# Dynamic convolution ahead of a two-layer product: channel blocks on partitions, and VectorE's 32x32 block turn in place of TensorE's transposes

## The chip, the cores and the metric

The kernel runs on one core of a Trainium2 chip. Its metric is the device time of one launch in microseconds (us), the median of three runs. Besides TensorE (PE; its weight loads are shown apart as PEld), VectorE (DVE), ScalarE (ACT), GpSimd (POOL) and SyncE (SP), the trace shows 16 DMA engines. Each engine works through its own instructions in order; semaphores are the only order between engines. TensorE's clock is shown as a share of its full speed.

## What is computed

```python
batch, seq, d_model = (4, 4096, 192)      # x: fp32
kernel_size, n_heads = 7, 8               # weight_gen: (4, 4096, 8, 7)
w = softmax(weight_gen, axis=-1)          # with + 1e-09 in the denominator
x_pad = concatenate([zeros(B, 6, D), x])  # six zero tokens ahead of each sequence
attn = einsum('bshk,bskhg->bshg', w, x_unf)   # seven taps per token and head, 24 channels a head
h = attn.reshape(16384, 192) @ w_in       # w_in: 192 x 2048
g = h * (1 / (1 + exp(-1.702 * h)))
out = g @ w_out                           # w_out: 2048 x 192
```

## The kernel before

**Precision.** Both products take fp32 values as a rounded part ("hi", type fp32r) and what is left of them ("lo"), so each fp32 product is three fp32r ones. The 192 rows of the first product are split into 128 "main" rows and 64 "rest" rows; the rest rows' hi and lo parts are stacked on 128 partitions (`xtr`), so one pass covers both. A 128-wide chunk of the hidden layer takes five matmuls of 512 columns (L474 to L479).

**Tiles.** Partition p holds the 128 tokens from 128p on. A tile takes 4 tokens of each partition (`TT = 4`), 512 tokens in all; there are 32 tiles. The first two and the last two tiles are written out, those between run in a loop of two tiles a turn (`over_tiles`). In each tile the 16 chunks are taken as 8 pairs, m = 0 to 7.

**One pair.** PE: `first_product` (10 matmuls into one of two `hid` slots in PSUM), then `second_product` of two pairs ago (`LAG = 2`, 16 matmuls into `acc`). ACT: `gate` (L268) and `gate_hi` (L271) from `hid`. DVE: `gate_lo` (L402), then the steps of the convolution of a coming tile that the table `CONV_AT` gives this pair. The second product of pair n waits for `gate_lo` of pair n; the first product of pair n waits for `gate_hi` of pair n-2, whose slot it writes.

**Convolution.** 18 steps on DVE: sum, add, reciprocal and product of the softmax on 128 x 32 and 128 x 224, then seven multiplications of 128 x 768 (L320) and six additions (L327; the last is split in `conv`, 128 x 512, and `conv_rest`, 128 x 256, L335). The window `xwin` holds 4 tokens and 6 tokens of halo. The first two windows' halo is loaded from the neighbouring partition's tokens in four DMAs of 31 partitions each (`first_window`, L188); later windows get theirs by an ACT copy from the window before (`carry_halo`, L255, at m = 3).

**Turning the tile.** The convolved tile has tokens on partitions and must have channels there. At m = 6 (`T_AT`) PE does six 128 x 128 transposes with the identity (L445, L448) into a `hid` slot. ACT then reads the rounded parts from it (L236, L238) and DVE the remainders (L371, L375).

**Start.** SP issues all loads in this order: the taps of three tiles, window 0 and its halos, the first layer in two halves of three DMAs, the identity, window 1 and its halos, the second layer, the remaining taps. DVE subtracts the maxima of the first taps, convolves tile 0, rounds the second layer (L365), splits tile 0 and then takes the second layer's remainder (L382). ACT rounds the first layer (L229, L230), POOL takes its remainders in four operations (L429). During tile 0 DVE takes four maxima of the remaining taps (L349), POOL subtracts each (L435), and in tile 1 ACT takes four exponentials, each with two table loads.

**End of a tile.** At m = 1 of the next tile ACT lifts one part of `acc` into `outs` (L248) and DVE adds the other (L391); `second_product` of m = 0 waits for that addition, part by part. SP stores `outs`.

Of the kernel before, what the change touches and what calls it, by code (L numbers as in the profile page):

```python
# [5 lines left out]
P = 128  # L22
# [5 lines left out]

TT = 4
LAG = 2  # L30
# [10 lines left out]
def ffn_of_dynamic_conv(nc: bass.Bass, x: bass.AP, weight_gen: bass.AP, w_in: bass.AP,  # L41
                        w_out: bass.AP, ident_dram: bass.AP, out: bass.AP):
    B, S, D = x.shape
    H, K = weight_gen.shape[2:]
    F = w_in.shape[1]
    GRP = D // H
    HALO = K - 1
    T = B * S // P
    TILES = T // TT
    NTOK = TT * P  # L50
    CH = F // P
    PAIRS = CH // 2
    STEPS = PAIRS + 1
    REST = D - P
    WIN = TT + HALO
    HK = H * K
    BATCH_P = P // B
    assert REST == 64 and NTOK == 512 and CH % 2 == 0 and TILES % BODY == 0 and (STEPS * BODY) % 2 == 0
    assert (BODY * PAIRS) % HI_SLOTS == 0 and S % T == 0


    FIRST_TILES = 3
    FIRST_TOKENS = FIRST_TILES * TT
    SHIFTS = 4
    STEP_TOKENS = (T - FIRST_TOKENS) // SHIFTS
    assert FIRST_TOKENS + SHIFTS * STEP_TOKENS == T
    HALVES = (slice(0, F // 2), slice(F // 2, F))
    TAP_PARTS = [(0, TT), (TT, FIRST_TOKENS)] + [(FIRST_TOKENS + i * STEP_TOKENS, FIRST_TOKENS + (i + 1) * STEP_TOKENS)
                                       for i in range(SHIFTS)]

    x_rows = x.rearrange("b s d -> (b s) d").rearrange("(p t) d -> p t d", t=T)
    out_rows = out.rearrange("b s d -> (b s) d").rearrange("(p t) d -> p t d", t=T) if len(out.shape) == 3 \
        else out.rearrange("(p t) d -> p t d", t=T)
    wg_rows = weight_gen.rearrange("b s h k -> (b s) (h k)").rearrange("(p t) c -> p (t c)", t=T)

    with ExitStack() as ctx:
# [5 lines left out]

# [9 lines left out]
        ident = sb("ident", [P, P])  # L92

        taps = sb("taps", [P, T * HK])
        tap_max = sb("tap_max", [P, T * H])
        tap_sum = sb("tap_sum", [P, TT * H])
        tap_inv = sb("tap_inv", [P, TT * H])
        tap_norm = sb("tap_norm", [P, TT * HK])
        xwin = sb("xwin", [P, 2, WIN, D])
        prod = sb("prod", [P, 2, TT * D])  # L100
        sums = sb("sums", [P, TT * D])
        conv = sb("conv", [P, 2, TT, P])
        conv_rest = sb("conv_rest", [P, 2, TT, REST])

        xt_hi = sb("xt_hi", [P, 2, NTOK], F32R)
        xt_lo = sb("xt_lo", [P, 2, NTOK], F32R)
        xtr = sb("xtr", [P, 2, NTOK], F32R)
# [21 lines left out]
        xt_raw = sem("xt_raw")  # L129
# [10 lines left out]
        def wait(eng, s, value):  # L140

            if not isinstance(value, int) or value > 0:
                eng.wait_ge(s, value)

        def over_tiles(eng, body):

            for j in range(BODY):
                body(j, j)
            with eng.Fori(1, TILES // BODY - 1) as it:
                for b in range(BODY):  # L150
                    body(it * BODY + b, b)
            for b in range(BODY):
                body(TILES - BODY + b, b)


        def pair_slot(b, m):
            return (b * STEPS + m + (m >= T_AT)) % 2

        def t_slot(b):
            return (b * STEPS + T_AT) % 2  # L160


        def rest_raw(s, e):
            return hid[e * REST:(e + 1) * REST, s, 1, 0:TT // 2 * P].rearrange("p (u n) -> p u n", n=P)

        def rest_of(xtr, lane, b, e):
            return xtr[lane:lane + REST, b, :].rearrange("p (u e n) -> p u e n", e=2, n=P)[:, :, e, :]

        HALO_LOADS = B
        def x_loads(j, b):  # L170

            return (1 + HALO_LOADS) * 16 + (j - b) * 8

        @block.sync
        def _(sp):
            n1 = FIRST_TOKENS * HK
            sp.dma_start(taps[:, 0:n1], wg_rows[:, 0:n1]).then_inc(taps_loaded[0], 16)

            def first_window(j):
                own = TT * (j + 1)
                sp.dma_start(xwin[:, j, WIN - own:WIN, :], x_rows[:, 0:own, :]).then_inc(x_loaded[j], 16)
                back = WIN - own
                for s in range(B):
                    lo = s * BATCH_P + 1
                    hi = (s + 1) * BATCH_P
                    sp.dma_start(xwin[lo:hi, j, 0:back, :],  # L188
                                 x_rows[lo - 1:hi - 1, T - back:T, :]).then_inc(x_loaded[j], 16)

            sp.wait_ge(halo_zero, 1)
            first_window(0)
            for h, f in enumerate(HALVES):
                sp.dma_start(w1_raw[:, f], w_in[0:P, f]).then_inc(w1_loaded[h], 16)
                sp.dma_start(w1r_raw[0:REST, f], w_in[P:D, f]).then_inc(w1_loaded[h], 16)
                sp.dma_start(w1r_raw[REST:P, f], w_in[P:D, f]).then_inc(w1_loaded[h], 16)
            sp.dma_start(ident[:], ident_dram).then_inc(const_loaded, 16)
            sp.wait_ge(halo_zero, 2)
            first_window(1)
            sp.dma_start(w2_raw[:], w_out.rearrange("(c p) d -> p c d", p=P)).then_inc(w2_loaded, 16)  # L200
            sp.dma_start(taps[:, n1:], wg_rows[:, n1:]).then_inc(taps_loaded[1], 16)

            def tile(j, b):

                if not isinstance(j, int) or j + 2 < TILES:
                    wait(sp, conv_ready, j + 1)
                    sp.dma_start(xwin[:, b, HALO:WIN, :], x_rows[:, bass.ds(TT * (j + 2), TT), :]
                                 ).then_inc(x_loaded[b], 16)

                wait(sp, evicted, TT * (j + 1))  # L210
                sp.dma_start(out_rows[:, bass.ds(TT * j, TT), :], outs[:, b, :, :]).then_inc(out_stored[b], 16)
# [6 lines left out]
        def _(act):  # L218
            def exponentials(part):
                act.wait_ge(taps_shifted, part + 1)  # L220
                lo, hi = TAP_PARTS[part]
                nc.scalar.activation(taps[:, lo * HK:hi * HK], taps[:, lo * HK:hi * HK], ACT.Exp
                                     ).then_inc(taps_exped, 1)

            exponentials(0)

            for h, f in enumerate(HALVES):
                act.wait_ge(w1_loaded[h], 48)
                nc.scalar.activation(w1_hi[:, f], w1_raw[:, f], ACT.Copy).then_inc(w1_hi_ready, 1)  # L229
# [311 lines left out]
```

## Time and profile before

| | us |
|---|---|
| median of three runs (1275.26 to 1276.52) | 1275.63 |
| span of the profiled execution, first to last instruction | 1272.1 |
| difference between the two, outside the span | 3.5 |
| busy TensorE, VectorE, ScalarE, GpSimd | 1209.2, 841.0, 621.3, 28.0 |

The profiled execution's own time is not listed apart from the three runs; its span is 3.5 us shorter than their median, and they differ by 1.3 us among themselves. All times in rows are us from the span's start, unless a column says ns. A matmul's duration in a row reaches past the start of the next, since they are pipelined: what one costs is the distance between starts. In the chain of waits, on the other hand, pieces don't overlap.

### The profile page before, as it was taken

What the parts mean: (1) busy time and instruction counts of PE and PEld (TensorE: products, weight loads), DVE (VectorE), ACT (ScalarE), POOL (GpSimd) and SP (SyncE); (2) the same over time, 40 slices, a digit from 0 to 9 for tenths busy, and PEclk for the clock granted to TensorE, in tenths of its full rate; (3) what the DMA queues carried; (4) which work ended last, traced back from release to release, by engine and by line L of the source; (5) the groups of instructions that cost most, each with busy time, mean ns of one, the idle gap of its engine ahead of it and who ended that gap; (6) DMA issues with size and microseconds to landing.
All of it is one profiled execution on the core that took longest, in us unless ns stands there. A gap on an engine that the chain in (4) does not pass through costs nothing.

```text
span 1272.1 us, 18060 instructions
## 1 busy us (share of the span) xinstructions
PE 1209.2 (95%) x6848; PEld 1095.6 (86%) x6848; DVE 841.0 (66%) x1066; ACT 621.3 (49%) x786; POOL 28.0 (2%) x14
## 2 busy tenths in 40 slices
PE   0398999999999999999999999999999999999998
PEld 0287899999999999999999999999999999999998
DVE  1997766666776666676666677666667666667732
ACT  0357644454454455454445445445545444544443
POOL 0321000000000000000000000000000000000000
PEclk9999999999999999999999999999999999999999
DMA  4400000000000000000000000000000000000000
GB/s 129 177 1 26 25 26 0 25 25 25 25 25 12 12 25 25 25 25 25 0 25 25 25 25 25 12 12 25 25 25 25 25 0 25 25 25 25 13 13 13
DMA packets 12590, 33.93 MB, mean 27 GB/s; under 512 B 1192, under 2 KB 3492, under 8 KB 12448
## 3 DMA queue, kind: packets, MB, share of 16 engines
q1 hardware_dynamic: 12576, 33.73, 8.0%
q8 instruction: 10, 0.16, 0.1%
q14 instruction: 4, 0.03, 0.0%
HBM read 21.14 MB, written 12.58 MB: 27 GB/s over the span
## 4 chain that ended last, share of the span: by engine, by line
PE 90%; DVE 6%; DMA 2%; ACT 1%; issue 0%; POOL 0%; SPq 0%; DVEq 0%; ACTq 0%; POOLq 0%
PE acc L494 30%; PE acc L496 14%; PE hid L474 9%; PE hid L478 9%; PE hid L476 9%; PE hid L475 9%; PE hid L479 9%; DMA xwin<-in_x 2%; DVE prod L320 2%; DVE sums L327 1%; PE hid L445 1%; DVE gate_lo L402 1%; DVE tap_max L349 1%; PE hid L448 1%; DVE conv_rest L335 0%
## 5 line engine op out<-in xcount | busy, mean ns | idle before, releaser
L494 PE MATMUL acc<-w,gate_hi 128*128 128x384 f32 x2048 | 603.7, 359 | 4.4 <-DVE outs L391 4.4
L402 DVE TENSOR_TENSOR gate_lo<-gate,gate_hi 128x1024 fp32r<-128x1024 f32 x256 | 314.5, 1228 | 373.0 <-ACT gate_hi L271 373.0
L268 ACT ACTIVATE gate<-hid 128x1024 f32<-128x1024 f32 x256 | 263.4, 1029 | 564.9 <-PE hid L479 564.8
L496 PE MATMUL acc<-w,gate_lo 128*128 128x192 f32 x2048 | 517.4, 253 | 0.0
L496 PEld LDWEIGHTS acc<-w,gate_lo 128*128 128x128 f32 x2048 | 391.4, 191 | 10.1
L494 PEld LDWEIGHTS acc<-w,gate_hi 128*128 128x128 f32 x2048 | 386.1, 189 | 15.7 <-DVE gate_lo L402 4.8
L271 ACT ACTIVATE gate_hi<-hid 128x1024 fp32r<-128x1024 f32 x256 | 261.5, 1021 | 0.0
L474 PE MATMUL hid<-xt_hi,w_hi 128*128 128x512 f32 x512 | 210.4, 411 | 3.1 <-DVE xtr L375 2.3
L478 PE MATMUL hid<-xtr,w1r_hi 128*128 128x512 f32 x512 | 203.8, 398 | 0.0
L475 PE MATMUL hid<-xt_lo,w_hi 128*128 128x512 f32 x512 | 201.9, 394 | 0.0
L476 PE MATMUL hid<-xt_hi,w_lo 128*128 128x512 f32 x512 | 201.7, 394 | 0.0
L479 PE MATMUL hid<-xtr,w1r_lo 128*128 128x512 f32 x512 | 201.3, 393 | 0.0
L320 DVE TENSOR_TENSOR prod<-xwin,tap_norm 128x768 f32<-128x768 f32 x192 | 188.7, 997 | 3.3
L327 DVE TENSOR_TENSOR sums<-sums,prod 128x768 f32<-128x768 f32 x160 | 156.5, 978 | 0.0
L479 PEld LDWEIGHTS hid<-xtr,w1r_lo 128*128 128x128 f32 x512 | 97.3, 190 | 21.9
L476 PEld LDWEIGHTS hid<-xt_hi,w_lo 128*128 128x128 f32 x512 | 96.7, 189 | 22.4
L478 PEld LDWEIGHTS hid<-xtr,w1r_hi 128*128 128x128 f32 x512 | 96.4, 188 | 22.5
L474 PEld LDWEIGHTS hid<-xt_hi,w_hi 128*128 128x128 f32 x512 | 96.8, 189 | 16.8 <-DVE xtr L375 3.4
L475 PEld LDWEIGHTS hid<-xt_lo,w_hi 128*128 128x128 f32 x512 | 97.6, 191 | 11.4
L445 PE MATMUL hid<-ident,conv 128*128 128x128 f32 x128 | 19.8, 278 | 51.9 <-DVE conv_rest L335 51.9
L445 PEld LDWEIGHTS hid<-ident,conv 128*128 128x128 f32 x128 | 14.6, 143 | 52.0 <-issue 51.7
L320 DVE TENSOR_TENSOR sums<-xwin,tap_norm 128x768 f32<-128x768 f32 x32 | 30.7, 958 | 25.4 <-DMA xwin<-in_x 24.0
(32 smaller groups left out, 364.3 us busy)
## 6 DMA issues: line engine op xcount, KB each, us to landing
out<-outs SPq DMA_DIRECT2D x32, 384.0 KB, 2.4
xwin<-in_x SPq DMA_DIRECT2D x31, 384.0 KB
taps<-in_weight_gen SPq DMA_DIRECT2D x1, 3248.0 KB, 19.5
w_raw<-in_moe_w_out SPq DMA_DIRECT2D x1, 1536.0 KB, 13.5
w_raw<-in_moe_w_in SPq DMA_DIRECT2D x2, 512.0 KB, 7.8
w1r_raw<-in_moe_w_in SPq DMA_DIRECT2D x4, 256.0 KB, 12.5
xwin<-in_x SPq DMA_DIRECT2D x1, 768.0 KB
xwin<-in_x SPq DMA_DIRECT2D x4, 139.5 KB
```

The costliest lines, as they stand in the source:

```text
L268: nc.scalar.activation(gate[:, m % 2, :], hid[:, s, :, :], ACT.Gelu_apprx_sigmoid).then_inc(gate_ready, 1)
L271: nc.scalar.activation(gate_hi[:, (b * PAIRS + m) % HI_SLOTS, :], hid[:, s, :, :], ACT.Gelu_apprx_sigmoid).then_inc(gate_hi_ready, 1)
L320: nc.vector.tensor_tensor(to.rearrange("p (g c) -> p g c", c=GRP), xwin[:, b, k:k + TT, :].rearrange("p t (h c) -> p (t h) c", c=GRP), tap ...
L327: nc.vector.tensor_tensor(sums[:], sums[:], prod[:, k % 2, :], ALU.add).then_inc(conv_op, 1)
L402: nc.vector.tensor_tensor(gate_lo[:, i, :], gate[:, m % 2, :], gate_hi[:, i, :], ALU.subtract).then_inc(gate_lo_ready, 1)
L474: nc.tensor.matmul(to, w1_hi[:, f], hi, start=True, stop=False)
L475: nc.tensor.matmul(to, w1_hi[:, f], lo, start=False, stop=False)
L476: nc.tensor.matmul(to, w1_lo[:, f], hi, start=False, stop=False)
L478: nc.tensor.matmul(to, w1r_hi[:, f], xtr[:, b, :], start=False, stop=False)
L479: last = nc.tensor.matmul(to, w1r_lo[:, f], xtr[:, b, :], start=False, stop=True)
L494: nc.tensor.matmul(acc[:, t, 0:2 * D], gate_hi[:, i, g], w2[:, c, :], start=(c == 0), stop=False)
L496: last = nc.tensor.matmul(acc[:, t, D:2 * D], gate_lo[:, i, g], w2[:, c, 0:D], start=False, stop=(c == CH - 1))
```

## The change

The host now lays out the inputs so that a partition holds one of four blocks of 48 channels of one of 32 runs of 512 tokens: partition 32q + r has block q of run r. Each run stands with its six tokens of halo in front. A tile takes 16 tokens of each run, again 512 tokens, so the convolution's operations keep their sizes (128 x 768, 128 x 224, 128 x 32), and the last addition is one operation of 128 x 768 in place of two. A window (22 tokens x 48 channels) comes with one DMA; there are no halo DMAs, no zeroing and no `carry_halo`.

DVE turns the convolved tile itself: two STREAM_TRANSPOSE operations of 128 x 512 in 32 x 32 blocks (`turn_tile`, at m = 4), SBUF to SBUF. The first gives the first 32 channels of each block, the second gives the remaining 16 twice. ACT rounds both (`round_tile`, after the gates of m = 5), and DVE takes the remainders (`split_tile`, at m = 5): a subtraction and an operation that multiplies by 0 or 1 and adds, which leaves hi on one half of the rows and lo on the other. The rows of the first layer are laid out alike on the host. PE has no transposes and no slot for them.

The first layer's first half is loaded by two DMAs that ACT issues; all else by SP, in smaller pieces and another order. The second layer is rounded in halves by ACT, and its remainders are taken by POOL. The output leaves in tile order and is put in order on the host.

```diff
-T_AT = 6
-HALO_AT = 3
-MAX_AT = (3, 4, 7, 7)
-EXP_AT = (0, 2, 4, 5)
-CONV_AT = (3, 3, 3, 2, 0, 0, 5, 2)
+TURN_AT = 4
+SPLIT_AT = TURN_AT + 1
+MAX_AT = (1, 2, 4, 6)
+EXP_AT = (0, 1, 3, 4)
+CONV_AT = (2, 2, 2, 2, 2, 3, 2, 2)
...
+            load_taps(0, 0, taps_loaded[0])
+            sp.dma_start(signs[:], sign_rows).then_inc(signs_loaded, 16)
+            for j in range(2):
+                sp.dma_start(xwin[:, j, :, :], x_runs[:, j * U:j * U + WIN, :]).then_inc(x_loaded[j], 16)
+            load_taps(1, 1, taps_loaded[1])
+            sp.dma_start(w2_raw[:, W2_HALVES[0], :], w2_rows[:, W2_HALVES[0], :]).then_inc(w2_loaded[0], 16)
+            sp.dma_start(w1_raw[:, HALVES[1]], w1_rows[:, HALVES[1]]).then_inc(w1_loaded[1], 16)
+            sp.dma_start(w1r_raw[:, HALVES[1]], w1r_rows[:, HALVES[1]]).then_inc(w1_loaded[1], 16)
+            sp.dma_start(w2_raw[:, W2_HALVES[1], :], w2_rows[:, W2_HALVES[1], :]).then_inc(w2_loaded[1], 16)
+            load_taps(2, 1 + SHIFTS, taps_loaded[2])
...
+            act.dma_start(w1_raw[:, HALVES[0]], w1_rows[:, HALVES[0]]).then_inc(w1_loaded[0], 16)
+            act.dma_start(w1r_raw[:, HALVES[0]], w1r_rows[:, HALVES[0]]).then_inc(w1_loaded[0], 16)
...
+            def round_tile(j, b):
+                wait(act, turned_ready, 2 * j + 2)
+                wait(act, hid_ready, PAIRS * (j - 1))
+                nc.scalar.activation(xt[:, b, 0, :], turned[:, 0, :], ACT.Copy).then_inc(xt_hi_ready, 1)
+                nc.scalar.activation(rest_hi[:], turned[:, 1, :], ACT.Copy, scale=signs[:, 0:1]
+                                     ).then_inc(xt_hi_ready, 1)
+            exponentials(0)
+            act.wait_ge(signs_loaded, 16)
+            round_w1(0)
+            round_w2(0)
+            round_w1(1)
+            round_tile(0, 0)
+            exponentials(1)
+            round_w2(1)
...
+            def turn_tile(j):
+                wait(dve, conv_ready, j + 1)
+                main, rest = (turned[:, i, :].rearrange("p (t u i) -> p u t i", t=TT, i=GROUPS) for i in range(2))
+                nc.vector.transpose(main, conv[:, :, 0:MAIN]
+                                    ).then_inc(turned_ready, 1)
+                nc.vector.transpose(rest, conv[:, :, MAIN:CB].unsqueeze(2).broadcast_to([P, U, 2, REST])
+                                    ).then_inc(turned_ready, 1)
+            def split_tile(j, b):
+                wait(dve, xt_hi_ready, 2 * j + 2)
+                nc.vector.tensor_tensor(xt[:, b, 1, :], turned[:, 0, :], xt[:, b, 0, :], ALU.subtract
+                                        ).then_inc(xt_lo_ready, 1)
+                nc.vector.scalar_tensor_tensor(xt[:, b, 2, :], turned[:, 1, :], signs[:, 1:2], rest_hi[:].bitcast(F32),
+                                               ALU.mult, ALU.add).then_inc(xt_lo_ready, 1)
...
-            def transposes(j, b):
-                s = t_slot((b + 1) % BODY)
-                wait(pe, conv_ready, j + 1)
-                for t in range(TT):
-                    nc.tensor.transpose(hid[:, s, 0, t * P:(t + 1) * P], conv[:, b, t, :], ident[:])
-                for t in range(0, TT, 2):
-                    last = nc.tensor.transpose(hid[:, s, 1, t // 2 * P:(t // 2 + 1) * P],
-                                               conv_rest[:, b, t:t + 2, :].rearrange("p t d -> p (t d)"), ident[:])
-                last.then_inc(xt_raw, 1)
```

On TensorE, before, at m = 6 of tile 0, with the last matmuls of pair 3's second product ahead and pair 6's first product behind:

```order
L494 MATMUL acc<-w,gate_hi 128x384
L496 MATMUL acc<-w,gate_lo 128x192
L445 MATMUL hid<-ident,conv 128x128 x4
L448 MATMUL hid<-ident,conv_rest 128x128 x2
L474 MATMUL hid<-xt_hi,w_hi 128x512
L475 MATMUL hid<-xt_lo,w_hi 128x512
```

The same place of the changed kernel:

```order
L411 MATMUL acc<-w,gate_hi 128x384
L413 MATMUL acc<-w,gate_lo 128x192
L392 MATMUL hid<-xt,w_hi 128x512
L393 MATMUL hid<-xt,w_hi 128x512
L394 MATMUL hid<-xt,w_lo 128x512
L395 MATMUL hid<-xt,w1r_hi 128x512
```

The second product now runs into the first with nothing between.

On VectorE, before, from the end of tile 0's convolution to the start of tile 1's, ahead of the first gate (w2 is the second layer):

```order
L335 TENSOR_TENSOR conv<-sums,prod 128x512
L335 TENSOR_TENSOR conv_rest<-sums,prod 128x256
L365 CAST w2<-w2_raw 128x16x192
L371 TENSOR_TENSOR xt_lo<-hid,xt_hi 128x512
L375 TENSOR_TENSOR xtr<-hid,xtr 64x2x128 x2
L382 TENSOR_TENSOR w2<-w2_raw,w2 128x16x192
L297 TENSOR_REDUCE tap_sum<-taps 128x32
```

The same stretch of the changed kernel:

```order
L274 TENSOR_TENSOR conv<-sums,prod 128x768
L297 STREAM_TRANSPOSE turned<-conv 128x4x4x32 [waits conv_ready]
L299 STREAM_TRANSPOSE turned<-conv 128x4x4x32
L286 TENSOR_REDUCE tap_max<-taps 128x64 [waits taps_loaded_second]
L291 TENSOR_TENSOR taps<-taps,tap_max 128x448 [waits taps_maxed]
L304 TENSOR_TENSOR xt<-turned,xt 128x512 [waits xt_hi_ready,signs_loaded]
L306 SCALAR_TENSOR_TENSOR xt<-turned,signs,rest_hi 128x512
L246 TENSOR_REDUCE tap_sum<-taps 128x32 [waits taps_exped]
```

The second layer's two operations have left VectorE, the two turns have come in, and the maxima and the shift of the second part of the taps stand behind the convolution instead of ahead of it.

On GpSimd, at the start of the changed kernel (`w` is the second layer there; before, it had two MEMSETs and the four operations on the first layer ahead of the taps):

```order
L357 TENSOR_TENSOR w_lo<-w_raw,w_hi 128x1024 [waits w1_hi_ready]
L357 TENSOR_TENSOR w1r_lo<-w1r_raw,w1r_hi 128x1024 [waits w1_hi_ready]
L362 TENSOR_TENSOR w<-w_raw,w 128x8x192 [waits w2_hi_ready]
L357 TENSOR_TENSOR w_lo<-w_raw,w_hi 128x1024 [waits w1_hi_ready]
L357 TENSOR_TENSOR w1r_lo<-w1r_raw,w1r_hi 128x1024 [waits w1_hi_ready]
L362 TENSOR_TENSOR w<-w_raw,w 128x8x192 [waits w2_hi_ready]
L374 TENSOR_TENSOR taps<-taps,tap_max 128x1624 [waits taps_maxed] x4
```

Two operations of 128 x 1536 on the second layer are new there.

## Rows read from the trace of the kernel before

**Rows 1.** The page: the span, and each engine's busy time

```profile
span 1272.1 us, 18060 instructions
PE 1209.2 (95%) x6848; PEld 1095.6 (86%) x6848; DVE 841.0 (66%) x1066; ACT 621.3 (49%) x786; POOL 28.0 (2%) x14
```

**Rows 2.** Busy time by stretch: one stretch in mid-kernel

```profile
600.00:640.00 40.00, 40.00 (x232) 36.40 (x231) 27.71 (x37) 21.13 (x27) 0.00 (x0) 1.00 0.11 36
```

**Rows 3.** TensorE in order of time (start, duration), around one tile's transposes

```profile
610.90 0.42 PE L474 MATMUL hid<-xt_hi,w_hi 128*128 128x512 f32 x1
...
615.52 0.60 PE L445 MATMUL hid<-ident,conv 128*128 128x128 f32 x4
...
616.10 0.48 PE L474 MATMUL hid<-xt_hi,w_hi 128*128 128x512 f32 x1
...
620.77 0.42 PE L474 MATMUL hid<-xt_hi,w_hi 128*128 128x512 f32 x1
```

**Rows 4.** Busy time by stretch, at the start and after a pause

```profile
2.00:4.00 2.00, 0.00 (x0) 0.00 (x0) 0.25 (x1) 0.02 (x1) 0.15 (x1) 1.00 0.85 235
8.00:10.00 2.00, 0.00 (x0) 0.00 (x0) 0.00 (x0) 0.00 (x0) 0.00 (x0) 1.00 0.06 25
105.00:110.00 5.00, 2.21 (x11) 2.25 (x11) 4.97 (x9) 4.95 (x5) 0.00 (x0) 0.84 0.15 59
```

**Rows 5.** The chain of waits in order of time (start, duration), up to tile 0

```profile
3.25 27.85 DMA xwin<-in_x
31.12 0.96 DVE sums L320
...
35.68 3.04 DVE sums L327
38.74 2.98 DVE prod L320
...
47.75 0.88 DVE sums L327
...
51.69 1.09 PE hid L445 x4
```

**Rows 6.** All engines in order of time, at the start

```profile
33.62 1.06 ACT L229 ACTIVATE w_hi<-w_raw 128x1024 fp32r<-128x1024 f32 x1 [28.63 <-DMA w1r_raw<-in_moe_w_in]
...
37.85 3.06 POOL L429 TENSOR_TENSOR w1r_lo<-w1r_raw,w1r_hi 128x1024 fp32r<-128x1024 f32 x1
...
55.52 0.79 PE L474 MATMUL hid<-xt_hi,w_hi 128*128 128x512 f32 x1 [2.32 <-DVE xtr L375]
```

**Rows 7.** The chain of waits again, tiles 0 and 1, to the pause's end

```profile
55.50 3.36 DVE w L382
...
78.07 3.19 DVE conv_rest L335
...
107.28 0.37 DVE outs L391
```

**Rows 8.** TensorE in order of time, at the pause

```profile
107.78 0.42 PE L494 MATMUL acc<-w,gate_hi 128*128 128x384 f32 x1 [4.37 <-DVE outs L391]
```

**Rows 9.** Groups by line: count, busy us, mean ns of one, idle before

```profile
L402 DVE TENSOR_TENSOR gate_lo<-gate,gate_hi 128x1024 fp32r<-128x1024 f32 x256 | 314.5, 1228 | 373.0 <-ACT gate_hi L271 373.0
L375 DVE TENSOR_TENSOR xtr<-hid,xtr 64x256 fp32r<-64x256 f32 x64 | 27.1, 423 | 2.0
L371 DVE TENSOR_TENSOR xt_lo<-hid,xt_hi 128x512 fp32r<-128x512 f32 x32 | 22.1, 691 | 13.5 <-ACT xt_hi L236 13.5
L335 DVE TENSOR_TENSOR conv<-sums,prod 128x512 f32<-128x512 f32 x32 | 21.9, 684 | 0.0
L236 ACT ACTIVATE xt_hi<-hid 128x512 fp32r<-128x512 f32 x32 | 19.1, 597 | 45.3 <-PE hid L448 45.3
L365 DVE CAST w<-w_raw 128x3072 fp32r<-128x3072 f32 x1 | 1.8, 1751 | 0.0
```

More of the change, by code:

```diff
@@ L27 @@
 AX_X = mybir.AxisListType.X
+QUADS = 4
+GROUPS = 32
+U = 16
 TT = 4
+MAIN = 32
 LAG = 2
-T_AT = 6
 HI_SLOTS = 4
 BODY = 2
-HALO_AT = 3
-MAX_AT = (3, 4, 7, 7)
-EXP_AT = (0, 2, 4, 5)
-CONV_AT = (3, 3, 3, 2, 0, 0, 5, 2)
[L41 to L51, printed above, removed]
-    PAIRS = CH // 2
[L53 to L59, printed above, removed]
+TURN_AT = 4
@@ L71, in ffn_of_dynamic_conv @@
[L71 to L74, printed above, removed]
+    W2_HALVES = (slice(0, CH // 2), slice(CH // 2, CH))
     with ExitStack() as ctx:
@@ L91, in ffn_of_dynamic_conv @@
         w2 = sb("w2", [P, CH, 2 * D], F32R)
[L92 to L107, printed above, removed]
+        taps = sb("taps", [P, RUN * HB * K])
+        tap_max = sb("tap_max", [P, RUN * HB])
+        tap_sum = sb("tap_sum", [P, G])
+        tap_inv = sb("tap_inv", [P, G])
+        tap_norm = sb("tap_norm", [P, N_TAP])
+        xwin = sb("xwin", [P, 2, WIN, CB])
+        prod = sb("prod", [P, 2, N_CONV])
+        sums = sb("sums", [P, N_CONV])
+        conv = sb("conv", [P, U, CB])
+        signs = sb("signs", [P, 2])
+        turned = sb("turned", [P, 2, NTOK])
+        rest_hi = sb("rest_hi", [P, NTOK], F32R)
+        xt = sb("xt", [P, 2, 3, NTOK], F32R)
         gate = sb("gate", [P, 2, 2 * NTOK])
@@ L153, in over_tiles, with last_tile @@
                 body(TILES - BODY + b, b)
[L156 to L172, printed above, removed]
+        def last_tile(j):
+            return isinstance(j, int) and j == TILES - 1
@@ L174, in _ @@
         @block.sync
         def _(sp):
[L176 to L199, printed above, removed]
@@ L405, in tile @@
                         evict(j - 1, (b + 1) % BODY)
-                    ahead = 1 if m < T_AT else 2
-                    start = sum(CONV_AT[:m]) + BEFORE if m < T_AT else sum(CONV_AT[T_AT:m])
-                    for part, at in enumerate(MAX_AT):
-                        if known and j == 0 and m == at:
-                            maxima(2 + part)
-                    if known and j + ahead >= TILES:
-                        continue
-                    for q in range(start, sum(CONV_AT[:m + 1]) + BEFORE if m < T_AT else sum(CONV_AT[T_AT:m + 1])):
-                        conv_step(dve, j + ahead, (b + ahead) % BODY, q)
+                    if known and j == 0 and m in MAX_AT:
+                        maxima(2 + MAX_AT.index(m))
+                    ahead = 1 if m < SPLIT_AT else 2
+                    if not (known and j + ahead >= TILES):
+                        first = BEFORE + sum(CONV_AT[:m]) if m < SPLIT_AT else sum(CONV_AT[SPLIT_AT:m])
+                        for q in range(first, first + CONV_AT[m]):
+                            conv_step(dve, j + ahead, (b + ahead) % BODY, q)
+                    if m == TURN_AT and not last_tile(j):
+                        turn_tile(j + 1)
+                    if m == SPLIT_AT and not last_tile(j):
+                        split_tile(j + 1, (b + 1) % BODY)
             over_tiles(dve, tile)
```

226 lines of the change are left out of this document (110 added, 116 removed).

## The prediction

> **What bounds the kernel now.** I read the page first: TensorE is busy for 1209.2 of 1272.1 us, VectorE for 841.0 and ScalarE for 621.3 [rows 1]. A mean can hide stages, so the busy time by stretch comes next: between 600 and 640 us TensorE is busy 40.00 of 40.00 us at full clock and VectorE 27.71 [rows 2]. So in mid-kernel TensorE's own instructions set the pace, and everything else has room. The table of idle time says the same from the other side: `gate_lo` on VectorE waited 373 us in all for ScalarE's gates [rows 9]. Two places are left where TensorE is not the bound. Ahead of its first product it does almost nothing until 55.52 us [rows 6], and there the chain of waits shows one long piece, a load of the window from 3.25 to 31.10 us, then VectorE's convolution of tile 0, then the transposes at 51.69 [rows 5]. And at 107.78 TensorE had stood still for 4.37 us, waiting for VectorE [rows 8], whose chain is unbroken from 55.50 to 107.28 [rows 7].
>
> **1. The transposes, 31 of 32.** In the order of TensorE, one pair starts at 610.90 and ends where the transposes start, 615.52: 4.62 us. The transposes and the next pair together take from 615.52 to 620.77: 5.25 us [rows 3]. So a tile's transposes, with the change between two streams of matmuls, cost 0.63 us on TensorE, though the six records read longer. The first of the 32 groups belongs to the start (part 2); 31 x 0.63 = 19.5 us go. Nothing takes their place on TensorE: the five matmuls a chunk keep their number and sizes. The work goes to engines with room. VectorE gets two turns of 128 x 512. No row shows such an operation; the nearest are `xt_lo`, 128 x 512, 0.69 us, and, cheaper per element, the cast of 128 x 3072 in 1.75 us, or 0.29 us for 512; dearer, `xtr`, 0.42 us for 256, or 0.85 us for 512 [rows 9]. I take 0.65 us each, nearest to the row of the same shape, 1.3 us a tile, and keep 0.6 to 1.7 for the pair. In exchange its split (0.69 + 2 x 0.42 = 1.5 us) becomes two operations of that shape, 1.3 us, and the last addition is one. VectorE's 841/32 = 26.3 us a tile become about 27.2, against a tile of 8 x 4.62 = 37.0 us. The dearest pair, m = 4, has a `gate_lo` of 1.2, two steps of 0.9 and the turns, 4.3 us: less than 4.62, so ScalarE finds the turned tile when it asks after the gates of m = 5, and the next tile's first product comes two pairs later. ScalarE loses the halo copy. I see no wait in mid-kernel. **-19.5 us.**
>
> **2. The start, up to the first product.** The load that ended last before was the halo's: in 8 to 10 us the DMA engines' mean share is 0.06, one of sixteen, at 25 GB/s, while at 2 to 4 us it is 0.85 and 235 GB/s [rows 4]. Four DMAs of 31 partitions and 139.5 KB each make 558 KB, which at 25 GB/s is 22 us: that is the long piece of the chain. They are gone; a window is now 128 rows of 4224 bytes. Window 0 (0.54 MB) shares the engines with the first taps (0.11 MB) and with what ScalarE issues (1.05 MB). If all of that must pass first, 1.70 MB at 235 GB/s are 7.2 us; from 2 us on this gives 9.2. I take 9, with 6 (served ahead of the weights) and 12 (at some 170 GB/s) as ends. The softmax of tile 0 is through by then.
>
> The Trainium skill speaks against the second queue as a gain: in "DMA: Bandwidth & Descriptors", section "Issuing engines are not separate DMA queues", DMAs that several engines issue run on the same 16 DMA engines and interleave, and only issue time is saved. By it the window is not served ahead of the weights, the late end above; without it the window would land at about 6, and the time would be 3 us less. No row of the kernel before shows two queues loading at once.
>
> Then the convolution of tile 0. Before, it ran from 31.12 to 51.55, 20.4 us. Four of its operations start 3.0 us apart rather than 0.9 (35.68 to 47.75: 12.1 us for what alone takes 3.7 [rows 5]), and in that stretch GpSimd has its four operations on the first layer, 3.06 us each [rows 6]. So each GpSimd operation of 128 x 1024 keeps VectorE out for 8.4/4 = 2.1 us, and the bare convolution is 20.4 - 8.4 = 12.0. **This is where the change gives back**: GpSimd has two more operations, of 128 x 1536, for the second layer, estimated at 1.5 x 2.1 = 3.1 us, and one of them falls among the steps of tile 0. By the rate above the second layer's first half has landed at 2 + 3.3/0.235 = 16 us, and the first layer's second half (4.3 MB) at 20, both within the convolution. So: 9 + 12.0 + 4 x 2.1 + 3.1 = 32.5.
>
> The Trainium skill has a rule for this ("SBUF — State Buffer", section "Who interferes with whom"): a VectorE operation with two SBUF inputs and a GpSimd operation that reads SBUF hold one port pair by turns, each for its whole length. The rows agree, with 3.0 us between starts in place of 0.9. A kernel in which the rule didn't hold would be through 11.5 us sooner.
>
> Then, in series: two turns 1.3, ScalarE's two roundings of 128 x 512 at 0.60 [rows 9] 1.2, VectorE's two remainders 1.3 (its maxima and shift of the second part of the taps, some 1.2 us, run beside ScalarE), and 0.1 for signals: 36.4 against 55.52. **-19.1 us.** Before, 4.0 us lay between the end of the convolution and the first product; now it is 3.9, so this exchange is worth nothing. Ends of the start: 32 (no window delay, or one GpSimd pair outside) and 42 (late loads, turns of 0.85).
>
> **3. Tile 0: VectorE is late.** Before, VectorE's unbroken chain from the first product to the first addition into `outs` is 107.28 - 55.50 = 51.8 us, and TensorE could have gone on 4.37 us earlier than 107.78, at 103.4, that is 47.9 after the first product [rows 7, 8]. Now VectorE has 3.4 less (the second layer's remainder, L382 [rows 7]), but the same remainder's second half on GpSimd, issued after ScalarE's rounding, may keep it out for 3.1; +1.3 for turns, -0.2 for the split, -0.2 for the joined addition, -0.9 for one step fewer ahead of that point. These come to -0.3. The four maxima are now at m = 1, 2, 4, 6, each with convolution steps right behind it. Each makes GpSimd shift 1624 columns. Before, two of them met steps and kept VectorE out for 2.8 us (`conv_rest`, 3.19 in place of 0.35 [rows 7]) and 4.1 for a pair, a third for 1.2: 8.1 us in all. Now all four can cost 2.8: 11.3, or +3.2. So VectorE needs 51.8 - 0.3 + 3.2 = 54.7 where TensorE needs 47.9 - 0.6 = 47.3: with 0.5 for the addition's way, a pause of 7.9 in place of 4.4, or **+3.5 us**, spread over some pairs. After the pause before, the granted clock was 0.84 [rows 4], between the two levels of 2.4 and 1.2 GHz; several pauses can do this more than once: **+1.0**. Ends: -2 (GpSimd finds VectorE at operations it doesn't hinder) and +9 (both two maxima's worth more and two further dips). The exponentials of tile 1 are one pair closer together; ScalarE falls behind by 1.6 us with each and recovers 2.5 in a free pair, which the two `hid` slots just cover. I count nothing.
>
> **The sum.** Span 1272.1 - 19.5 - 19.1 + 3.5 + 1.0 = 1238.0; with the 3.5 us outside the span, **1241.5 us**. The first load is the same fixed cost in both, and the last tile's end is unchanged.
>
> **The rivals.**
> *A. The window still lands late.* If something among the first loads is served as the halos were (the 8-byte rows of `signs` are ahead of it), the window comes at up to 31 us. GpSimd's work is then mostly done: 31 + 12 + 3 + 4 = 50, a gain of 5.5 at the start: 1255. For it: one slow DMA held back all others before. Against it: every DMA now covers 128 partitions, and such ones ran at 0.85 of the engines [rows 4]. 6 in 100.
> *B. The turns are dear, but covered.* With 2 to 4 us each (strided in and out), mid-kernel still has the room: VectorE 26 + 8 = 34 of 37 us. But tile 0 has none: twice up to 6 us more ahead of tile 1, 1247 to 1253. For it: no row shows the operation, and its views have four dimensions. Against it: `gate_lo` and `xtr` show 1.2 to 1.7 ns an element whatever their views [rows 9]. 8 in 100.
> *C. Slower than before.* VectorE becomes the bound in every tile. It has 26 us without the turns; it passes TensorE's 37 us from 5.5 us a turn, and the time before (37.6 a tile, plus the 18 us won at the start, 0.6 a tile) is reached from 6 us a turn. At 7 us a turn a tile takes 40, and the whole 1275 + 31 x 2.4 - 18 = 1331. The dearest row would have to be wrong by a factor of seven: 3 in 100.
> *D. Tile 0 gives the start's gain back.* VectorE is the bound through both, so an earlier first product would only wait longer behind it: 1272.1 - 19.5 + 3.5 = 1256. Against it: the 28 us of waiting for the load were idle time of VectorE too, and its own added work is under 10 us. 3 in 100.
>
> **How the numbers follow.** The forecast's case has 80 in 100, the rivals the 20 above. The range takes the ends of parts 2 and 3 against each other, not all at once: from a start at 32 and a tile 0 as before, 1272.1 - 19.5 - 23.5 + 0 + 3.5 = 1232.6, to a start at 42 and a tile 0 of +7, 1272.1 - 19.5 - 13.5 + 7 + 3.5 = 1249.6. With part of B it is 1232 to 1251. About 0.2% (2.5 us) is what a measurement of this kernel tells from no change. Faster: 0.96; within: 0.01; slower: 0.03.
>
> **What would show it.** On TensorE, eight starts of `first_product` a tile at 4.62 us, with no gap at m = 6, and a tile of 37.0 us. Window 0 ends the wait of the first multiplication at 6 to 12 us. Five GpSimd operations lie over the convolution of tile 0, with steps 3 us apart, and the first product starts near 36. Turns of about 0.65 us, and in mid-kernel no idle TensorE. In tile 0, idle TensorE behind `gate_lo` of pairs 2 to 7 and at the first addition, 8 us in all. I am wrong if the turn takes over 2 us, if a wait for `turned` or `xt` comes back in every tile, or if the start is outside 32 to 42.

## The result, and the profile after

The changed kernel takes 1236.59 us (median of four runs, 1236.57 to 1236.64), the kernel before in the same comparison 1275.66 (four runs, 1275.26 to 1276.52). The ratio is 0.9694, with a 95% interval of 0.968 to 0.9707. The profiled execution took 1236.58 us with a span of 1234.8.

The page of the changed kernel, for [rows 1]:

```profile
span 1234.8 us, 17474 instructions
PE 1189.4 (96%) x6656; PEld 1071.5 (87%) x6656; DVE 876.8 (71%) x1064; ACT 588.4 (48%) x726; POOL 34.2 (3%) x14
```

TensorE has 192 instructions less and is still busy for nearly the whole span; VectorE has 36 us more and ScalarE 33 less. The busy time by stretch answers [rows 2] and [rows 4] (stretch, its length, then busy us of PE, PEld, DVE, ACT and POOL, granted clock, share of the DMA engines, GB/s):

```profile
8.00:10.00 2.00, 0.00 (x0) 0.00 (x0) 1.50 (x2) 1.39 (x2) 1.48 (x1) 1.00 1.03 416
75.00:80.00 5.00, 5.00 (x21) 4.56 (x20) 4.89 (x7) 2.96 (x4) 0.78 (x1) 0.66 0.00 0
600.00:640.00 40.00, 40.00 (x228) 36.21 (x227) 27.57 (x35) 19.36 (x24) 0.00 (x0) 1.00 0.07 23
```

Where one DMA engine of sixteen moved 25 GB/s between 8 and 10 us, all of them now move 416. In mid-kernel TensorE is without a gap, as before. Behind a pause in tile 0 TensorE's granted clock was 0.66 of full speed over 5 us, and 0.50, its lower level of 1.2 GHz, from 76 to 78 us.

TensorE in mid-kernel, where a new pair begins at the rows' start times, for [rows 3]:

```profile
606.50 0.41 PE L392 MATMUL hid<-xt,w_hi 128*128 128x512 f32 x1
...
611.13 0.41 PE L392 MATMUL hid<-xt,w_hi 128*128 128x512 f32 x1
```

That is 4.63 us a pair, 4.627 over a long stretch, and from 93 us on no pair is longer.

The chain of waits up to the first product and across tile 0 (start, duration), for [rows 5] and [rows 7]:

```profile
1.67 6.80 DMA xwin<-in_x_runs
8.50 0.96 DVE sums L266
9.46 6.04 DVE prod L266 x2
15.49 4.11 DVE sums L271
...
25.65 0.96 DVE prod L266
...
35.60 0.66 DVE xt L306
...
50.05 3.70 DVE prod L266
...
90.18 0.28 DVE outs L324
```

The window lands at 8.5 in place of 31.1. From then on most of the multiplications and additions come 3 to 4 us apart until 25.65, when GpSimd's fifth operation has ended, and 0.9 us apart from there. That fifth operation, from all engines in order of time:

```profile
21.75 3.05 POOL L357 TENSOR_TENSOR w1r_lo<-w1r_raw,w1r_hi 128x1024 fp32r<-128x1024 f32 x1
```

TensorE's first product and all its waits behind it, the last at the first addition, for [rows 6] and [rows 8] (in brackets the idle time before):

```profile
36.32 0.79 PE L392 MATMUL hid<-xt,w_hi 128*128 128x512 f32 x1 [36.32 <-DVE xt L306]
...
62.41 0.44 PE L411 MATMUL acc<-w,gate_hi 128*128 128x384 f32 x1 [2.57 <-DVE gate_lo L333]
...
74.19 0.44 PE L411 MATMUL acc<-w,gate_hi 128*128 128x384 f32 x1 [2.27 <-DVE gate_lo L333]
...
90.59 0.42 PE L411 MATMUL acc<-w,gate_hi 128*128 128x384 f32 x1 [0.66 <-DVE outs L324]
```

The groups by line with the new operations, for [rows 9]:

```profile
L297 DVE STREAM_TRANSPOSE turned<-conv 128x512 f32<-128x512 f32 x32 | 22.8, 712 | 1.1
L299 DVE STREAM_TRANSPOSE turned<-conv 128x512 f32<-128x512 f32 x32 | 21.4, 669 | 0.0
```

Cut at these rows, the span's change of 37.3 us has three pieces. The first product starts 19.2 us earlier (36.3 in place of 55.5). From there to the second product of tile 0's end that waits for the first addition, 52.3 us have become 54.3: 2.0 longer. From there to the end it is 20.1 us shorter (1144.2 in place of 1164.3).

### The profile page after: what moved, and what is told of

The parts are those of the page before. It is cut to its first block, busy times and chain, and to the rows that moved or that the text cites. A ratio compares the mean times of both kernels' runs of the same rounds, so it can differ in the third digit from the quotient of the medians.

```text
span 1234.8 us, 17474 instructions
## 1 busy us (share of the span) xinstructions
PE 1189.4 (96%) x6656; PEld 1071.5 (87%) x6656; DVE 876.8 (71%) x1064; ACT 588.4 (48%) x726; POOL 34.2 (3%) x14
## 4 chain that ended last, share of the span: by engine, by line
PE 92%; DVE 7%; DMA 1%; ACT 0%; issue 0%; SPq 0%; DVEq 0%
PE acc L411 31%; PE acc L413 15%; PE hid L392 10%; PE hid L393 9%; PE hid L395 9%; PE hid L394 9%; PE hid L396 9%; DVE prod L266 2%; DVE sums L271 1%; DVE gate_lo L333 1%; DVE tap_max L286 1%; DMA xwin<-in_x_runs 1%; DVE sums L266 0%; DVE conv L274 0%; DVE tap_norm L255 0%; DVE turned L297 0%
## 5 line engine op out<-in xcount | busy, mean ns | idle before, releaser
L392 PE MATMUL hid<-xt,w_hi 128*128 128x512 f32 x512 | 209.1, 408 | 36.3 <-DVE xt L306 36.3
L393 PE MATMUL hid<-xt,w_hi 128*128 128x512 f32 x512 | 204.7, 400 | 0.0
L395 PE MATMUL hid<-xt,w1r_hi 128*128 128x512 f32 x512 | 203.0, 396 | 0.0
L394 PE MATMUL hid<-xt,w_lo 128*128 128x512 f32 x512 | 202.8, 396 | 0.0
L396 PE MATMUL hid<-xt,w1r_lo 128*128 128x512 f32 x512 | 201.7, 394 | 0.0
L392 PEld LDWEIGHTS hid<-xt,w_hi 128*128 128x128 f32 x512 | 96.5, 189 | 47.1 <-DVE xt L306 36.3
L395 PEld LDWEIGHTS hid<-xt,w1r_hi 128*128 128x128 f32 x512 | 96.6, 189 | 24.7
L396 PEld LDWEIGHTS hid<-xt,w1r_lo 128*128 128x128 f32 x512 | 97.5, 190 | 23.1
L394 PEld LDWEIGHTS hid<-xt,w_lo 128*128 128x128 f32 x512 | 96.6, 189 | 23.3
L393 PEld LDWEIGHTS hid<-xt,w_hi 128*128 128x128 f32 x512 | 97.8, 191 | 11.8
L324 DVE TENSOR_TENSOR outs<-acc,outs 128x192 f32<-128x192 f32 x128 | 36.9, 348 | 2.9 <-ACT outs L208 2.8
L208 ACT ACTIVATE outs<-acc 128x192 f32<-128x192 f32 x128 | 32.6, 358 | 3.9 <-PE acc L413 3.9
## 6 DMA issues: line engine op xcount, KB each, us to landing
w_raw<-in_w_rows SPq DMA_DIRECT2D x2, 768.0 KB, 10.2
```

The source lines that it names most:

```text
L392: nc.tensor.matmul(to, w1_hi[:, f], hi, start=True, stop=False)
L393: nc.tensor.matmul(to, w1_hi[:, f], lo, start=False, stop=False)
L394: nc.tensor.matmul(to, w1_lo[:, f], hi, start=False, stop=False)
L395: nc.tensor.matmul(to, w1r_hi[:, f], rest, start=False, stop=False)
L396: last = nc.tensor.matmul(to, w1r_lo[:, f], rest, start=False, stop=True)
```

## The experiments

Each is an edit of the changed kernel unless it says otherwise, and its time stands against 1236.59. The kernel before ran beside all of them, with medians of 1274.7, 1275.0 and 1275.5.

**1. TensorE's transposes put back.**

```diff
+            def spare_transposes(j, m):
...
+                wait(pe, gate_hi_ready, j * PAIRS + m - 1)
+                for e, k in ((0, 0), (0, 1), (0, 2), (0, 3), (1, 0), (1, 1)):
+                    nc.tensor.transpose(hid[:, m % 2, e, k * P:(k + 1) * P], w1_raw[:, k * P:(k + 1) * P],
+                                        ident[:])
...
+                    if m == 6 and not last_tile(j):
+                        spare_transposes(j, m)
```

> The changed kernel with six 128x128 transposes put back on TensorE ahead of pair 6's first product in 31 tiles; they read constant weights and write a slot of hid that the first product overwrites, so nothing uses them. Theory (a tile's transposes cost TensorE 0.63 us and nothing else of the gain in mid-kernel depends on them): 31 x 0.63 = 19.5 us more, 1256. Rival (part of the old cost was the waiting for and reading of the turned tile, not the matmuls): clearly less, about half, 1246.

Measured: 1255.89 us (1255.78 to 1255.98), 19.3 more. TensorE in order of time, from one tile's transposes to the end of the pair behind them:

```profile
634.18 0.82 PE L425 MATMUL hid<-ident,w_raw 128*128 128x128 f32 x6
...
639.45 0.42 PE L395 MATMUL hid<-xt,w_hi 128*128 128x512 f32 x1
```

Transposes and pair together take 5.27 us, for 5.25 in [rows 3], and a tile 0.64 us more than in the changed kernel. Times 31 that is 19.8 us; the 0.5 us that are missing lie ahead of tile 2, where TensorE waits for VectorE anyway. The term of 19.5 us is right, and it was the matmuls themselves: these transposes wait for nothing that VectorE makes.

**2. GpSimd writes zeros.**

```diff
-                    nc.gpsimd.tensor_tensor(lo[:, HALVES[h]], raw[:, HALVES[h]], hi[:, HALVES[h]], ALU.subtract
-                                            ).then_inc(w1_lo_ready, 1)
+                    nc.gpsimd.memset(lo[:, HALVES[h]].bitcast(F32), 0.0).then_inc(w1_lo_ready, 1)
...
-                nc.gpsimd.tensor_tensor(w2[:, W2_HALVES[h], D:2 * D], w2_raw[:, W2_HALVES[h], :],
-                                        w2[:, W2_HALVES[h], 0:D], ALU.subtract).then_inc(w2_lo_ready, 1)
+                nc.gpsimd.memset(w2[:, W2_HALVES[h], D:2 * D].bitcast(F32), 0.0).then_inc(w2_lo_ready, 1)
```

> GpSimd writes zeros in place of the six remainders of both layers' weights, so those lo parts are left out of the products; the number and place of its operations stay. Theory (a GpSimd operation that reads SBUF keeps a two-input VectorE operation out for its whole length): the convolution of tile 0 has its 12.0 us again, the first product starts near 25 in place of 36.3, and 3 us less are lost in tile 0: 1236.6 - 11.3 - 3 = 1222. Rival (the steps 3 to 4 us apart come from the loads, which run at over 400 GB/s in the same stretch): no change at the start, 1236.

Measured: 1224.54 us (1224.19 to 1225.06), 12.0 less, where 14.3 were expected. All engines in order of time show GpSimd's operations on the weights in their old order, each now 0.95 or 1.38 us long in place of 3.1 to 4.1, and the chain of waits shows what VectorE does beside them:

```profile
9.67 0.95 POOL L357 MEMSET w1r_lo<- 128x1024 f32 x1
...
16.20 0.95 POOL L357 MEMSET w_lo<- 128x1024 f32 x1 [0.72 <-ACT w_hi L180]
```

```profile
8.84 0.96 DVE sums L266
9.80 1.74 DVE prod L266 x2
11.54 0.88 DVE sums L271
...
18.98 0.88 DVE sums L271
19.88 0.97 DVE conv L274
...
29.64 1.02 ACT gate L216
30.66 0.93 ACT gate_hi L219
31.61 1.23 DVE gate_lo L333
```

The convolution takes 12.0 us, from 8.84 to 20.85, with the same loads under way (467 GB/s between 15 and 20 us, 471 in the changed kernel), and the first product starts at 24.96, 11.4 us earlier. So the loads don't slow VectorE; GpSimd's subtractions do. GpSimd's writes alone don't: no step of VectorE beside a MEMSET is longer than alone. It is what the Trainium skill says in "SBUF — State Buffer", section "SBUF: two separate sides": a VectorE operation with two SBUF inputs contends only with a GpSimd operation that reads SBUF.

The 3 us expected in tile 0 did not come. There the sixth subtraction had kept VectorE out for 2.9 us (the `tap_norm` of 3.27 at 37.20). Without it VectorE waits 2.6 us for ScalarE's gate of pair 0, and its first `gate_lo` starts 6.65 us behind the first product, hardly sooner than before (6.94).

**3. First loads from one queue.**

```diff
-            for j in range(2):
-                sp.dma_start(xwin[:, j, :, :], x_runs[:, j * U:j * U + WIN, :]).then_inc(x_loaded[j], 16)
+            sp.dma_start(xwin[:, 0, :, :], x_runs[:, 0:WIN, :]).then_inc(x_loaded[0], 16)
+            sp.dma_start(w1_raw[:, HALVES[0]], w1_rows[:, HALVES[0]]).then_inc(w1_loaded[0], 16)
+            sp.dma_start(w1r_raw[:, HALVES[0]], w1r_rows[:, HALVES[0]]).then_inc(w1_loaded[0], 16)
+            sp.dma_start(xwin[:, 1, :, :], x_runs[:, U:U + WIN, :]).then_inc(x_loaded[1], 16)
...
-            act.dma_start(w1_raw[:, HALVES[0]], w1_rows[:, HALVES[0]]).then_inc(w1_loaded[0], 16)
-            act.dma_start(w1r_raw[:, HALVES[0]], w1r_rows[:, HALVES[0]]).then_inc(w1_loaded[0], 16)
```

> All first loads from SP: first taps, signs, window 0, the first layer's first half, window 1, then as before. Theory (one set of 16 engines serves both queues, and ScalarE's loads only take bandwidth from window 0): window 0 lands by 6, the multiplications start when the softmax is through, at 7.2 in place of 8.5, and the weights come 1 us later with the same number of GpSimd operations over the convolution: 1235.3. Rival (the second queue brings bandwidth or issue time that the start needs): same or slower, 1236.6 to 1239.

Measured: 1233.79 us (1233.49 to 1233.95), 2.8 less, with the first product at 33.7. The gain is twice what I expected. I had taken the softmax's end at 7.2 us as given, but the first taps also shared the engines with ScalarE's loads. Here they are in the changed kernel, and then in this one, all engines in order of time:

```profile
4.51 0.39 DVE L286 TENSOR_REDUCE tap_max<-taps 128x32 f32<-128x224 f32 x1 [4.51 <-DMA taps<-in_tap_runs]
```

```profile
2.84 0.39 DVE L286 TENSOR_REDUCE tap_max<-taps 128x32 f32<-128x224 f32 x1 [2.84 <-DMA taps<-in_tap_runs]
...
5.97 0.96 DVE L266 TENSOR_TENSOR sums<-xwin,tap_norm 128x768 f32<-128x768 f32 x1 [0.45 <-DMA xwin<-in_x_runs]
...
9.09 1.06 ACT L180 ACTIVATE w_hi<-w_raw 128x1024 fp32r<-128x1024 f32 x1 [5.02 <-DMA w1r_raw<-in_w1r_rows]
```

The taps are there 1.7 us and the window 2.5 us earlier, and the weights, which nothing early waits for, 1.7 us later. The part of the change that lets ScalarE issue the first layer's first half is a loss of 2.8 us.

**4. No shifts on GpSimd.**

```diff
-                nc.gpsimd.tensor_tensor(t, t, tap_max[:, lo * HB:hi * HB].unsqueeze(2).broadcast_to(t.shape),
-                                        ALU.subtract).then_inc(taps_shifted, 1)
+                nc.gpsimd.memset(idle[:, part:part + 1], 0.0).then_inc(taps_shifted, 1)
```

> GpSimd's four subtractions of the maxima from the later taps are left out (it writes two idle columns instead); the softmax is the same without them for these inputs. Theory (each keeps VectorE out for 2.8 us, and VectorE sets the pace of tile 0): 11.1 us less for VectorE up to the first addition, TensorE's lateness there of 7.0 us goes to about 0: 1229.6. Rival (the lateness comes from the four maxima and the order of VectorE's steps): 2 us or less, above 1234.

Measured: 1225.99 us (1225.47 to 1226.41), 10.6 less, 3.6 more than the theory gives. TensorE's waits after the first product shrink to one of 0.6 us, and pair 16 begins at 109.15 in place of 116.08: 6.9 us, the expected 7.0. The rest came later: a pair took 4.613 us in mid-kernel in place of 4.627. Nothing of GpSimd runs there. What was different there was `idle`, a new tile of 24 bytes a partition, which moved the tiles declared after it.

**5. That tile alone.**

```diff
         signs = sb("signs", [P, 2])
+        idle = sb("idle", [P, 6])
```

> The changed kernel with an unused tile of 24 bytes a partition declared behind signs, which moves the tiles declared after it, nothing else. In the kernel without GpSimd's shifts, which had such a tile, a pair took 4.613 us in mid-kernel, in all others 4.627. Theory (the address of a tile that TensorE reads sets those 14 ns): 4.613 a pair, 250 x 0.014 = 3.5 us less, 1233. Rival (it came from GpSimd's part): 4.627 and 1236.6.

Measured: 1233.32 us (1233.30 to 1233.45), 3.3 less, and 4.613 us a pair. In mid-kernel, in order of time:

```profile
609.82 0.41 PE L393 MATMUL hid<-xt,w_hi 128*128 128x512 f32 x1
...
614.43 0.41 PE L393 MATMUL hid<-xt,w_hi 128*128 128x512 f32 x1
```

So the addresses of the tiles behind `signs`, among them `xt` and the gates that TensorE reads, are worth 14 ns a pair. `signs` has 8 bytes a partition, the first tile of the kernel whose size isn't a multiple of 32; with `idle` the two come to 32. Tiles of 512 and 2048 bytes at the same place (experiments 1 and 6) leave the rate at 4.627. Which address and which tile it is wasn't tried.

**6. More turns.** Three more in each tile, and then twenty:

```diff
+                for i in range(3):
+                    wait(dve, spare_turned, j * 3 + i)
+                    nc.vector.transpose(spare[:].rearrange("p (t u i) -> p u t i", t=TT, i=GROUPS), conv[:, :, 0:MAIN]
+                                        ).then_inc(spare_turned, 1)
```

> Three more turns of 128x512 into an unused tile in every tile, between the two that count: some 2.0 us more for VectorE and for the tile's path to TensorE. Theory (the turns are hidden in mid-kernel and stand in the open only at the start and in tile 0): 2.0 us at the start and 2.0 in tile 0, nothing a tile later: 1240.6. Rival (ScalarE's wait for the turned tile reaches TensorE in each tile): 1 us or more a tile, above 1265.

Measured: 1240.99 us (1240.70 to 1241.10), 4.4 more, with the first product at 38.7 (2.4 later, of which the three turns are 2.1) and 4.627 us a pair in mid-kernel. ScalarE now waits for the turned tile in each tile (86.7 us in 32 waits, from 25.5 in two), and none of it reaches TensorE. VectorE's turns cost nothing in mid-kernel, and their price stands in the open twice, at the start and in tile 0.

> Twenty more turns in every tile, 13.2 us at 0.66 each: VectorE has 27.4 + 13.2 = 40.6 us a tile where TensorE has 37.0. Theory (VectorE's sum a tile decides): a tile of 41 us, TensorE idle 4 us in each, in all 30 x 3.7 + 13 at the start + 13 in tile 0 = 137 us more, 1374. Rival (the long piece between two gates decides by itself, since ScalarE waits behind it with the gates of the next pairs): a tile of 44 us or more, above 1450.

Measured: 1592.47 us, one run. A tile takes 48.1 us (the last turn's starts, 47.9 to 1539.1, in 31 steps). VectorE is busy for 41.3 us a tile (1320.4 in 32), some 42 with the short gaps between turns, so its sum doesn't decide: it still waits 226 us for gates. The waits of TensorE and the chain in one tile, then the stretch:

```profile
PE acc L417 <- DVE gate_lo L339: 274.5, 32, 15.5
```

```profile
711.98 0.68 DVE spare L303
...
727.43 1.12 DVE gate_lo L339
728.59 0.69 PE acc L417
```

```profile
725.00:735.00 10.00, 6.41 (x25) 6.04 (x26) 9.83 (x15) 4.89 (x6) 0.00 (x0) 0.60 0.00 0
```

From the `gate_lo` of m = 4, at 708.23, to that of m = 5 are 19.2 us, and TensorE, which needs the latter two pairs after its gate, stands still for 8.6 us a tile; behind each pause its clock is lower (0.60 of full speed in that stretch), which by subtraction makes up the rest of the 11 us. Of the two expectations the rival holds.

**7. The kernel before with its halos spread.**

```diff
-                for s in range(B):
-                    lo = s * BATCH_P + 1
-                    hi = (s + 1) * BATCH_P
+                for lo, hi in ((16, P), (1, 16)):
                     sp.dma_start(xwin[lo:hi, j, 0:back, :],
                                  x_rows[lo - 1:hi - 1, T - back:T, :]).then_inc(x_loaded[j], 16)
```

> The kernel before, with each window's halo loaded by two DMAs of 112 and 15 partitions in place of four of 31; the first six tokens of three sequences then read the end of the sequence before in place of zeros. Theory (a DMA of 31 partitions is served by one engine, and that alone held the start): window 0 lands near 8, the convolution runs 8 + 12 + 8.4, and the first product starts near 32 in place of 55.5: 1251. Rival (the queue itself, or the order of the loads, held the window): it lands after 20, above 1262.

Measured: 1251.70 us (1251.05 to 1252.50), 23.3 less than the kernel before beside it. This kernel leaves out the zeros ahead of three of the four sequences; what restoring them would cost wasn't tried. The chain of waits and the busy time by stretch:

```profile
2.69 5.94 DMA xwin<-in_x
8.65 0.96 DVE sums L318
...
33.03 3.36 DVE w L380
```

```profile
6.00:8.00 2.00, 0.00 (x0) 0.00 (x0) 1.07 (x4) 0.00 (x0) 0.00 (x0) 1.00 0.94 255
```

Nearly the same bytes (127 partitions in place of 124) land at 8.6 in place of 31.1, at 0.94 of the engines in place of 0.06, and the first product starts at 33.1. It was the DMAs' 31 partitions. The Trainium skill has the rule in "DMA: Bandwidth & Descriptors", section "Why a DMA increments its semaphore by 16 and not by 1": a DMA uses the largest number of engines up to 16 that divides the slowest dimension of both its sides; by it 31 partitions get 1 engine, 112 get 16 and 15 get 15. But for those zeros, the start was to be had without turning the layout, and 3.3 us better than in the changed kernel: four GpSimd operations lie over this convolution (20.4 us), five over that one (23.7).

**8. GpSimd's work on VectorE.**

```diff
             turn_tile(0)
+            rest_w1(0, 0)
+            dve.wait_ge(signs_loaded, 16)
+            split_tile(0, 0)
+            rest_w1(0, 1)
             maxima(1)
             shift(1)
-            dve.wait_ge(signs_loaded, 16)
-            split_tile(0, 0)
+            rest_w2(0)
...
+                    if known and j == 0 and m == 0:
+                        rest_w1(1, 0)
+                        rest_w1(1, 1)
+                    if known and j == 0 and m == 2:
+                        rest_w2(1)
                     if known and j == 0 and m in MAX_AT:
                         maxima(2 + MAX_AT.index(m))
+                        shift(2 + MAX_AT.index(m))
```

> The changed kernel with GpSimd's ten operations (six remainders of weights, four shifts of taps) done by VectorE itself; those that aren't needed for the first product stand behind it, in tile 0. Theory (an operation on GpSimd costs VectorE more than doing it itself: 2.1 against 1.1 us for 128x1024, 2.8 against 1.7 for 1624 columns): the convolution of tile 0 runs bare, 8.5 + 12, and the first product starts near 26 in place of 36.3; tile 0 gets 14 us of work in place of 14 us of being kept out, so it stays as late as it is: 1226. Rival (what VectorE takes over costs it what the waiting did): 1234 or more.

Measured: 1226.77 us (1226.62 to 1226.83), 9.8 less, the first product at 25.99. The chain of waits:

```profile
41.02 1.85 DVE taps L291
42.87 0.88 DVE sums L271
43.75 0.02 issue
43.77 0.96 DVE prod L266
...
79.24 1.14 DVE gate_lo L347
```

A shift costs VectorE 1.85 us by its own hand and 2.7 by GpSimd's (3.70 for a multiplication in place of 0.96). Added up from the rows of both kernels: GpSimd's ten operations kept VectorE out for 11.7 us in the convolution, 2.9 at `tap_norm` and 10.9 in four shifts, 25.5 in all; by its own hand they take it 4 x 1.14, 2 x 1.67 and 4 x 1.85, 15.3 us. The difference of 10.2 is near the 9.8 measured. Where they stand decides too: only one of the six weight remainders now lengthens the way to the first product. The two effects weren't run apart.

**9. The three gains together.** Experiments 3, 5 and 8 in one kernel.

> The same with the first loads from SP alone (window 0 ahead of the weights) and the unused tile of 24 bytes. Theory (the three gains are of separate places and add up): window 0 at 6.0, the first product near 23.7, tile 0 as late as before, 4.613 us a pair: 1226 - 2.5 - 3.4 = 1220. Rival (with an earlier start the weights' loads and roundings or the later taps become late): the first product after 26 or new waits for loads, 1223 or more.

Measured: 1220.69 us (1220.55 to 1220.78), a ratio of 0.9571 to the kernel before (0.9555 to 0.9587), and 15.9 us less than the changed kernel. TensorE's first product, and the chain at the start:

```profile
23.10 0.77 PE L388 MATMUL hid<-xt,w_hi 128*128 128x512 f32 x1 [23.10 <-DVE w1r_lo L313]
```

```profile
1.67 4.05 DMA xwin<-in_x_runs
5.74 0.96 DVE sums L267
...
21.82 1.14 DVE w1r_lo L313
```

The sum of the single gains is 2.8 + 3.3 + 9.8 = 15.9: they add up, within the few tenths by which executions differ.

## Why the prediction was right, point by point

**The bound.** Right: TensorE in mid-kernel, VectorE at the start and in tile 0. Adding to VectorE (experiment 6) and taking from it (2, 4, 8) moved the time only by what happened in those two places, but for the 3.6 us in 4 that a tile's address made; only twenty added turns reached TensorE in mid-kernel.

**The transposes, -19.5.** Right, 19.3 by experiment 1. In the result 1.7 us of it are hidden: the changed kernel's pair takes 4.627 us and the old one's 4.62, over 240 pairs. The step "the five matmuls a chunk keep their number and sizes" was true and not enough: addresses changed too, and by experiment 5 they can move a pair by 14 ns. That they made these 7 is not shown.

**The turns.** 0.71 and 0.67 us for the assumed 0.65, near the row of the same shape, 0.69. They are hidden in mid-kernel, as forecast.

**The start, -19.1.** Measured -19.2. The parts were right too: the window at 8.5 for 9, the convolution's end at 32.2 for 32.5 with five GpSimd operations over it, then 4.1 us for 3.9. The side remark that the second queue costs 3 us rather than winning any was right, 2.8 by experiment 3, but it counted the window alone, and the first taps were late too.

**Tile 0, +3.5.** TensorE reaches the product that waits for the first addition 54.3 us after its start, where 47.3 would do: 7.0 late, for 7.9. The pause didn't come at one place; TensorE stood still for 2.6 and 2.3 us for `gate_lo` and then 0.7, and its clock fell after the second, which accounts for the rest. The steps beside the four shifts are 2.7 us longer each (3.70 in place of 0.96), and experiment 4, which leaves the shifts out, gets the 7 us back.

**The clock, +1.0.** This term is what failed, together with the next one. For the stretch from the pause's end on, the sum had 30 of the 31 transposes, -18.9, and +1.0 for the clock: -17.9. Measured is -20.1, so the term had the wrong sign, -1.2 in place of +1.0. The lower clock in tile 0 is already inside the 7.0, and the old kernel's own slow stretch went away: behind its long pause the second product from 107.78 on took 3.8 us, to the next first product, in place of 2.3, and the clock there was low [rows 4]:

```profile
111.58 0.55 PE L474 MATMUL hid<-xt_hi,w_hi 128*128 128x512 f32 x1
```

The tiles' steady gain, 30 x (37.59 - 37.01), is 17.4 of the 20.1. Of the other 2.7, 1.5 are this second product, and 1.1 are the old kernel's transposes of tile 1 with the pair behind them, which from 125.6 on took 6.4 us in place of 5.25, 0.6 of it a wait for ScalarE's `gate_hi`. The forecast had kept both in the kernel after.

**The time outside the span, +3.5.** It measured 1.8 in every execution, of the kernel before as well: its executions of 1273.99 and 1275.43 us have spans of 1272.2 and 1273.6. I had set the span of one short execution against the median of others. The kernel before varies by 2.7 us between executions, and the one profiled, by its span, was at the low end. That is 1.7 of the 4.9 us by which the forecast was too high; the start (0.1), the pause (0.9) and the stretch behind it (2.2) are the others. All four erred to the same side, so the range held by its width, not by errors that cancel.

**The rivals.** A (the window late) and D (tile 0 gives all back) did not come. B and C needed dear turns. C's mechanism was wrong as I wrote it: I let VectorE's sum a tile decide, from 6 us a turn, but by experiment 6 the piece between two gates decides first. With 14.8 us added, a tile took 48.1 us where the sum would give some 42.

## What to carry to other kernels

An engine that is free in the mean can be the bound at the start and in the first tile, where all one-time work meets: cost each edit there by itself, since a saving on the steady bound and a saving of idle time at the start are separate sums. Ask of work given to GpSimd what it keeps VectorE from; here VectorE lost more time to GpSimd's operations (25.5 us) than it needed to do them itself (15.3). And look at the number of partitions of each early DMA, before turning a layout round.

## What I had not expected of the hardware

- An added tile of 24 bytes a partition, used by nothing, took 3.3 us off: 4.613 us a pair in place of 4.627.
- Loads of 1 MB issued by a second engine delayed the first taps, a load of 0.11 MB, from 2.84 to 4.51 us.
- The executions of the kernel before lie between 1273.8 and 1276.5 us, those of the changed one within 0.1. Experiment 7, which keeps the old layout, varies by 1.5. Experiment 1, with transposes in the new one, varies by 0.2, so TensorE's transposes alone don't explain it. Nor does the layout: experiments 2 and 4, in the new one, vary by 0.9. What does stays open.
